# Attention into two feed-forward layers on one core: another order of the front's turns, the first weight blocks later, the eleventh unit pooled later

## The chip, the core and the metric

The kernel runs on one core of a Trainium2 chip. TensorE (PE) does the matrix products, VectorE (DVE), ScalarE (ACT) and GpSimd (POOL) the element-wise work, and SyncE (SP) issues most of the DMAs. The five engines run their own instruction lists in order and wait for each other through semaphores. The metric is the device time of one launch in microseconds (us), lower is better.

## The reference, cut to what matters

```python
# q, k, v: batch 4, heads 8, seq 576, head_dim 64
k_p = k.reshape(B, H, Sp, 8, D).mean(axis=3)         # keys and values pooled by 8
v_p = v.reshape(B, H, Sp, 8, D).mean(axis=3)
scores = scale * np.matmul(q, k_p.transpose(0, 1, 3, 2))
attn = softmax(scores)                               # over the 72 pooled keys
x = (attn @ v_p) as (2304 tokens, 512)
x = f1(x @ w_in) @ w_out                             # 512 -> 2048 -> 512, f1 a piecewise square
x = softplus(x @ w2_in) @ w2_out                     # the same sizes
```

## The kernel before

The attention is cut into 16 units, one for a pair of heads of a batch entry. The first ten (0 to 9, `FIRST = 10`) are done in the front, before the feed-forward layers; the other six are spread over the first products of layer 1. The products of the layers run in fp32r with each operand split into a high and a low part, three matmuls for each block. The rest of the program, from about 76 us on, is a nearly unbroken row of these matmuls on PE.

A unit passes through these steps in the front, and the text uses the short names on the left:

- **TQ(u)** on PE: six transposes of q (L1155) and two small matmuls that transpose and pair the keys (L1161), into PSUM banks 0 and 1. ACT then copies qT and kT out (`copy_qk`, L652 and L655). There is one qT and one kT buffer, so the copy of unit u waits until the scores of all units before u are done (`wait(act, scored, 2 * u)`).
- **S(u)** on PE: ten matmuls for the scores (L1178). DVE takes maxima and subtracts them (`take_max` L911, `shift` L918), ACT takes the exponential (`exp_scores` L661).
- DVE sums the exponentials (L934), inverts the sums (L939) and multiplies (L946): the softmax weights of unit u.
- **TP(u)** on PE: two groups of five transposes of the weights, h = 0 and h = 1 (L1199). ACT copies each group out (`copy_p`, L668 and L669). The group h = 1 of unit u waits until the results of all units before u have been stored (`wait(pe, x_stored, u)`), since it uses the same PSUM bank.
- **A(u)** on PE: the product with v (L1215). It waits for the weights' copies and for `v_summed`, the last pooling step of v on DVE (`sum_v`, L899). ACT stores the result in X (`store_x`, L674).
- POOL does the other pooling steps of k and v (`pool_keys` L553 and L559, `pool_values` L538 and L541).

Each engine's program is written out by hand as a loop over turns. In turn i of the front PE does S(i+1), TQ(i+2), A(i-2), TP(i-1), in this order; ACT does `copy_qk(i+2)`, `store_x(i-2)`, then the copies of TP(i-1) and the exponentials of unit i+1. DVE's turn i (`turn` in the vector block) is: sums of unit i, maxima of unit i+1 with the inversion of the sums between them, the two subtractions for unit i+1, weights of unit i, and last `sum_v(i-1)`.

After turn 8 PE does A(7), TP(8), A(8), TP(9) and A(9), and between them the first two blocks of layer 1's product, `make_h(0, 0)` and `make_h(0, 1)`, which are made in four chunks c0 to c3 of six matmuls each (L1263). The chunk c needs piece c of X split into high (ACT, L744) and low part (POOL L594 for pieces 0 and 1, DVE L992 for 2 and 3), and the weight block 0 split likewise (`hi_w` on ACT, L759; `lo_w(0, 0)` on POOL, L601). The third block, `make_h(0, 2)`, begins at 76.04 us in the profiled execution; from there on PE hardly waits.

SP loads k, q and v of each unit (288 KB each) and, between them, the weight blocks (`load_weights`, L439).

Of the kernel before, what the change touches and what calls it, by code (L numbers as in the profile page):

```python
# [38 lines left out]
FIRST = 10  # L39
# [23 lines left out]
PIECES = 4  # L63
# [22 lines left out]
LATE = FIRST - 2  # L86
# [4 lines left out]
def build(nc, q, k, v, w1_in, w1_out, w2_in, w2_out, out):  # L91
    with ExitStack() as ctx:
# [66 lines left out]
        def k_of(u):  # L159
            return k_one[:, 0, 4 * HD:6 * HD]  # L160
# [127 lines left out]
        def fill_done(n, piece):  # L288

            if n == 0:  # L290
                return (fill_lo_pool, piece + 1) if piece < FIRST_BY_POOL else (fill_lo_dve, piece - FIRST_BY_POOL + 1)
            if n in LO_BY_POOL:
                return fill_lo_pool, FIRST_BY_POOL + PIECES * LO_BY_POOL.index(n) + piece + 1
            before = n - 1 - sum(1 for m in LO_BY_POOL if m < n)
            return fill_lo_dve, PIECES - FIRST_BY_POOL + PIECES * before + piece + 1
# [113 lines left out]
        def _(sp):  # L409

            def load_k(u):
                wait(sp, k_paired, u - 3)
                sp.dma_start(k_in(u), k_src[u]).then_inc(k_loaded[u % PAIRS], 16)
# [17 lines left out]
            def load_weights(layer, k):  # L431

                n, slot = layer * JJ + k, W_ORDER[layer][k]
                if k >= 2:
                    sp.wait_ge(*w_done(layer, W_ORDER[layer][k - 2]))
                elif layer == 1:
                    sp.wait_ge(t_added, 4)
                for f in range(2):
                    sp.dma_start(w_raw[:, n % 2, f, :].rearrange("p (c j) -> p c j", c=KC),  # L439
                                 win_src[layer][slot + JJ * f]).then_inc(w_loaded[n % 2], 16)  # L440
# [43 lines left out]
            for u in range(3, FIRST):  # L484
                load_k(u)
                load_q(u)
                load_v(u - 2)
                if u >= LATE:
                    load_weights(0, u - LATE)
            for u in range(FIRST - 2, FIRST):  # L490
                load_v(u)
            load_shared(FIRST)
            load_weights(0, 2)
# [32 lines left out]
        def _(pool):  # L526
# [22 lines left out]
            def pool_keys(u):  # L549
                x = k_in(u)  # L550
                if u < FIRST:
                    pool.wait_ge(k_loaded[u % PAIRS], 16 * (u // PAIRS + 1))
                    nc.gpsimd.tensor_tensor(x[:, :, 0:4 * HD], x[:, :, 0:4 * HD], x[:, :, 4 * HD:8 * HD],  # L553
                                            ALU.add).then_inc(k_halved, 1)
                    pool.wait_ge(k_halved, u + 1)
                    wait(pool, qk_transposed, u - 1)
                    two, one = (x[:, :, r * 2 * HD:(r + 1) * 2 * HD].rearrange("p h (r d) -> p h r d", r=2)
                                for r in range(2))
                    nc.gpsimd.tensor_tensor(k_pair[:, u % 2, :, :].rearrange("p r (h d) -> p h r d", h=2), two, one,  # L559
                                            ALU.add).then_inc(k_paired, 1)  # L560
                else:
                    pool_sums(u, k_in(u), (k_one_loaded, 16 * (u - FIRST + 1)), k_halved, k_paired)
                    last_sum(u, k_in(u), k_of(u).rearrange("p (h d) -> p h d", h=2), k_paired, k_pooled)

            def pool_values(u):
                if u < FIRST:
                    pool_sums(u, v_in(u), (v_loaded[u % PAIRS], 16 * (u // PAIRS + 1)), v_halved, v_paired)
                else:
                    pool_sums(u, v_in(u), (v_one_loaded, 16 * (u - FIRST + 1)), v_halved, v_paired)
                    last_sum(u, v_in(u), v_in(u)[:, :, 0:HD], v_paired, v_pooled)  # L570
# [19 lines left out]
            def fill_lo_piece(n, piece):  # L590

                pool.wait_ge(fill_hi, PIECES * n + piece + 1)
                (data, source), = x_parts(n, piece)
                nc.gpsimd.tensor_tensor(xs[n % 2][:, 1, data], source, xs[n % 2][:, 0, data].bitcast(F32),  # L594
                                        ALU.subtract).then_inc(fill_lo_pool, 1)

            def lo_w(layer, k):

                n, slot = layer * JJ + k, W_ORDER[layer][k]
                pool.wait_ge(w_hi, n + 1)  # L600
                nc.gpsimd.tensor_tensor(W[:, slot, :, 1, :], w_raw[:, n % 2, :, :], W[:, slot, :, 0, :].bitcast(F32),  # L601
                                        ALU.subtract).then_inc(w_lo_pool, 1)
# [16 lines left out]
                                        ).then_inc(s_added, 1)  # L619

            pool_values(FIRST - 3)
            lo_w(0, 0)
            pool_values(FIRST - 2)
            fill_lo_piece(0, 0)
            pool_values(FIRST - 1)
            fill_lo_piece(0, 1)
            pool_keys(FIRST)
            pool_values(FIRST)
            for layer in range(2):
# [13 lines left out]
        def _(act):  # L643
# [19 lines left out]
            def copy_p(u, h):  # L663

                bank = p_bank(u, h)
                act.wait_ge(p_transposed, 2 * u + h + 1)
                a = NS_A * SSTEP
                nc.scalar.activation(pT_of(u, h)[:, 0:a], ps[0:SP, bank, 0:a], ACT.Copy)  # L668
                nc.scalar.activation(pT_of(u, h)[:, a:S], ps[0:SP, bank + 1, 0:S - a], ACT.Copy).then_inc(p_copied, 1)  # L669
# [8 lines left out]
            def turn(i):  # L678

                if i <= FIRST - 3:  # L680
                    copy_qk(i + 2)
                if 2 <= i:
                    store_x(i - 2)
                if 6 <= i < 6 + PIECES:
                    fill_hi_piece(0, i - 6)
                for h in range(2):
                    if 1 <= i <= FIRST:
                        copy_p(i - 1, h)
                    if i <= FIRST - 2:
                        exp_scores(i + 1, h)  # L690
                if 5 <= i < 7:
                    hi_w(0, i - 5)

            def load_shared_qk(u):

# [51 lines left out]
            def hi_w(layer, k):  # L747

                n, slot = layer * JJ + k, W_ORDER[layer][k]
                act.wait_ge(w_loaded[n % 2], 32 * (n // 2 + 1))  # L750
                if layer == 0 and slot >= 3:
                    act.wait_ge(x_stored, FIRST)
                elif layer == 1 and slot in (2, 3):
                    act.wait_ge(step_done, 6 * NT)
                elif layer == 1 and slot >= 4:
                    act.wait_ge(t_lo, 2 * PRODUCTS)
                elif layer == 1:
                    act.wait_ge(step_done, STEPS)
                nc.scalar.activation(W[:, slot, :, 0, :], w_raw[:, n % 2, :, :], ACT.Copy).then_inc(w_hi, 1)  # L759
# [80 lines left out]
            for layer in range(2):  # L840
# [32 lines left out]
                for m in range(1, STEPS + 2):  # L873
# [6 lines left out]
                    p, i = divmod(m - 2, NT)  # L880
# [261 lines left out]
        def _(pe):  # L1142
# [75 lines left out]

            def turn(i):

                if i <= FIRST - 2:
                    score(i + 1)
                if i <= 0:
                    keep_warm(WARM[i + 1])
                if i <= FIRST - 3:
                    transpose_qk(i + 2)
                if 2 <= i:
                    attend(i - 2)
                if i >= 1:
                    for h in range(2):  # L1230
                        transpose_p(i - 1, h)

# [16 lines left out]
            def make_h(layer, a, chunks=range(KC)):  # L1249

                k, f = divmod(a, 2)
                n, fill, slot = layer * HPAIRS + a, fill_of(layer, k // JJ), W_ORDER[layer][k % JJ]
                banks, x = bank_pair(v_of_pair[n]), xs[fill % 2]
                for c in chunks:
                    if c == 0:
                        pe.wait_ge(*w_done(layer, slot))
                        pe.wait_ge(*banks_free(v_of_pair[n]))
                    if a % (2 * JJ) == 0:
                        pe.wait_ge(*fill_done(fill, c))
                    for s, (part, x_part) in enumerate(((0, 0), (1, 0), (0, 1))):  # L1260
                        for tb in range(2):
                            at = c * PIECE + tb * TB
                            last = mm(banks[:, tb, :], W[:, slot, f, part, c * P:(c + 1) * P], x[:, x_part, at:at + TB],  # L1263
                                      start=c == 0 and s == 0, stop=c == KC - 1 and s == 2)
                if KC - 1 in chunks:
                    last.then_inc(h_done, 1)
# [80 lines left out]
            make_h(0, 0, (2,))  # L1347
            for h in range(2):
                transpose_p(FIRST - 1, h)
            make_h(0, 1, (1,))  # L1350
            attend(FIRST - 1)
            make_h(0, 0, (3,))
            make_h(0, 1, (2, 3))
            for layer in range(2):
                for a in range(2 if layer == 0 else 0, HPAIRS):
                    make_h(layer, a)
# [32 lines left out]
```

## Time and profile before

| what | us |
|---|---|
| median of 3 timed runs | 867.46 (866.34 to 874.46) |
| profiled execution, own time | 862.46 |
| its span, first to last instruction | 860.7 |
| one turn of the front (36.18 to 41.05) | 4.87 |
| last scores of the front, S(9), end | 55.28 |
| `make_h(0, 2)` begins | 76.04 |

The span is 1.76 us shorter than the execution's own time, and the profiled execution is 5.0 us shorter than the median of the timed runs. PE is busy for 98% of the span, DVE for 69%, ACT for 57%, POOL for 42%. The page gives the busy time of each engine and the clock granted to PE in 40 slices of 21.5 us; the clock has two levels here, 2.4 GHz (1.00) and 1.2 GHz (0.50).

### The profile page before, as it was taken

To read this page: it belongs to the slowest core of one execution; us is meant where nothing else is said; L and a number is where in the kernel's file an instruction comes from. 1 tells how busy PE (TensorE), PEld (TensorE's weight loads), DVE (VectorE), ACT (ScalarE), POOL (GpSimd) and SP (SyncE) were. 2 spreads that over 40 slices of the span, in tenths; PEclk is the share of its full clock that TensorE was granted. 3 is DMA by queue.
4 is the path that set the end of the run, shared out by engine and by line. 5 is a ranking of instruction groups with operands and counts; after the bars stand their busy time and mean duration, and the time that the engine had idled before them with its cause. 6 is when DMAs were issued, how large, how long until landed. Compare 5 with 4: busy or idle time off the path is not lost.

```text
span 860.7 us, 13035 instructions
## 1 busy us (share of the span) xinstructions
PE 845.8 (98%) x5198; PEld 822.7 (96%) x5198; DVE 592.0 (69%) x618; ACT 490.5 (57%) x700; POOL 360.8 (42%) x290
## 2 busy tenths in 40 slices
PE   8989999999999999999999999999999899999998
PEld 7768999999999999999999999999999899999998
DVE  4983855532233598768657698898899989778642
ACT  3875665644445453444435868978887654445442
POOL 6994677744454600000000498888766500000000
PEclk9979999999999999999999999999999999999999
DMA  8952767565555896454633235675655698645532
GB/s 195 209 126 78 209 209 230 185 220 188 181 183 188 274 395 224 167 220 154 227 109 99 96 123 189 211 243 182 211 200 176 204 397 306 239 164 203 200 113 73
DMA packets 106539, 167.82 MB, mean 195 GB/s; under 512 B 21872, under 2 KB 94448, under 8 KB 101872
## 3 DMA queue, kind: packets, MB, share of 16 engines
q1 hardware_dynamic: 93800, 157.86, 54.9%
q10 hardware_dynamic: 12680, 9.14, 3.7%
q8 instruction: 41, 0.67, 0.3%
q14 instruction: 18, 0.15, 0.1%
HBM read 96.21 MB, written 70.78 MB: 194 GB/s over the span
## 4 chain that ended last, share of the span: by engine, by line
PE 84%; DVE 6%; ACT 3%; DMA 3%; SPq 1%; issue 1%; POOL 1%; ACTq 0%; DVEq 0%
PE ps L1263 41%; PE ps L1281 37%; DVE t_a L1052 2%; DMA ops<-gops 2%; PE ps L1178 1%; DVE ops L1064 1%; PE ps L1215 1%; DMA w_raw<-in_moe_w_in_dram 1%; PE ps L1296 1%; PE ps L1321 1%; PE ps L1199 1%; DVE xs L992 1%; ACT qT L652 1%; PE ps L1155 1%; DVE t_a L1055 1%
## 5 line engine op out<-in xcount | busy, mean ns | idle before, releaser
L1263 PE MATMUL ps<-xs,W 128*128 128x384 f32 x2304 | 408.2, 336 | 0.8 <-DVE ops L1044 0.8
L1263 PEld LDWEIGHTS ps<-xs,W 128*128 128x128 f32 x2304 | 399.3, 188 | 5.8 <-issue 4.9
L1281 PE MATMUL ps<-xs,Tm 128*128 128x384 f32 x1968 | 345.9, 336 | 3.4 <-DVE xs L992 3.0
L1281 PEld LDWEIGHTS ps<-xs,Tm 128*128 128x128 f32 x1968 | 342.2, 189 | 4.3 <-issue 3.5
L744 ACT ACTIVATE xs<-ops 128x768 fp32r<-128x768 f32 (+1 forms) x148 | 111.7, 826 | 159.1 <-PE ps L1281 149.9
L608 POOL TENSOR_TENSOR ops<-ops 128x384 f32<-128x384 f32 x48 | 72.9, 1519 | 303.2 <-DVE ops L1064 221.9
L992 DVE TENSOR_TENSOR xs<-ops,xs 128x768 fp32r<-128x768 f32 (+1 forms) x148 | 130.2, 941 | 1.8 <-ACT xs L744 1.8
L1044 DVE SCALAR_TENSOR_TENSOR ops<-ps,t_a 128x768 f32<-128x768 f32 x48 | 45.9, 956 | 110.4 <-ACT t_a L768 110.2
L766 ACT ACTIVATE t_a<-ps 128x768 f32<-128x768 f32 x48 | 39.0, 812 | 96.2 <-PE ps L1263 96.2
L1077 DVE TENSOR_TENSOR X<-ps,X 128x768 f32<-128x768 f32 x41 | 38.7, 955 | 77.8 <-PE ps L1281 77.8
L1064 DVE TENSOR_TENSOR ops<-t_a,t_b 128x768 f32<-128x768 f32 x48 | 62.8, 1308 | 19.7 <-ACT t_b L787 17.9
L1052 DVE SCALAR_TENSOR_TENSOR t_a<-t_b,t_a 128x768 f32<-128x768 f32 x48 | 71.4, 1487 | 1.1 <-ACT t_b L782 1.1
L618 POOL TENSOR_TENSOR ops<-ops 128x384 f32<-128x384 f32 x48 | 63.7, 1327 | 3.8
L615 POOL TENSOR_TENSOR ops<-ops 128x384 f32<-128x384 f32 x48 | 64.1, 1335 | 0.0
L610 POOL TENSOR_TENSOR ops<-ops 128x384 f32<-128x384 f32 x48 | 56.1, 1170 | 0.0
L775 ACT ACTIVATE t_a<-ps 128x768 f32<-128x768 f32 x48 | 38.8, 809 | 30.0 <-DVE ops L1064 24.7
L787 ACT ACTIVATE t_b<-t_b 128x768 f32<-128x768 f32 x48 | 40.2, 838 | 12.5 <-DVE t_a L1052 12.5
L1055 DVE SCALAR_TENSOR_TENSOR t_a<-ps,t_a 128x768 f32<-128x768 f32 x48 | 46.0, 958 | 1.7
L744 ACT ACTIVATE xs<-X 128x768 fp32r<-128x768 f32 x46 | 37.4, 836 | 10.9 <-PE ps L1281 7.1
L992 DVE TENSOR_TENSOR xs<-X,xs 128x768 fp32r<-128x768 f32 x36 | 40.7, 1155 | 1.9 <-ACT xs L744 1.9
L777 ACT ACTIVATE t_a<-t_a 128x768 f32<-128x768 f32 x48 | 40.7, 848 | 1.6
L768 ACT ACTIVATE t_a<-t_a 128x768 f32<-128x768 f32 x48 | 40.6, 847 | 1.5
(88 smaller groups left out, 650.6 us busy)
## 6 DMA issues: line engine op xcount, KB each, us to landing
gops<-ops SPq DMA_DIRECT2D x48, 1344.0 KB, 5.8
ops<-gops SPq DMA_DIRECT2D x36, 1536.0 KB, 6.8
X<-gops SPq DMA_DIRECT2D x22, 384.0 KB, 6.4
w_raw<-in_moe_w_in_dram SPq DMA_DIRECT2D x32, 256.0 KB, 3.9
t_raw<-in_moe_w_out_dram SPq DMA_DIRECT2D x6, 1024.0 KB, 10.0
out_dram<-y_out ACTq DMA_DIRECT2D x11, 384.0 KB, 2.6
k_raw<-in_k_dram SPq DMA_DIRECT2D x10, 288.0 KB
q_raw<-in_q_dram SPq DMA_DIRECT2D x20, 144.0 KB, 7.6
```

The source lines that it names most:

```text
L608: nc.gpsimd.tensor_tensor(ops[:, slot, S1, :], ops[:, slot, G21, :], ops[:, slot, G22, :], ALU.add).then_inc(s_added, 1)
L610: nc.gpsimd.tensor_tensor(ops[:, slot, S3, :], ops[:, slot, G11, :], ops[:, slot, G21, :], ALU.subtract).then_inc(s_added, 1)
L615: nc.gpsimd.tensor_tensor(ops[:, slot, S2, :], ops[:, slot, S1, :], ops[:, slot, G11, :], ALU.subtract).then_inc(s_added, 1)
L618: nc.gpsimd.tensor_tensor(ops[:, slot, S4, :], ops[:, slot, G12, :], ops[:, slot, S2, :], ALU.subtract).then_inc(s_added, 1)
L744: last = nc.scalar.activation(xs[n % 2][:, 0, data], source, ACT.Copy)
L992: last = nc.vector.tensor_tensor(xs[n % 2][:, 1, data], source, xs[n % 2][:, 0, data].bitcast(F32), ALU.subtract)
L1044: nc.vector.scalar_tensor_tensor(out=g, in0=bank_pair(v_of_pair[a]), scalar=1.0, in1=t_a[:, a % 2, :, :], op0=ALU.max, op1=ALU.min).then_i ...
L1052: nc.vector.scalar_tensor_tensor(out=u, in0=b, scalar=1.0, in1=u, op0=ALU.subtract, op1=ALU.subtract).then_inc(r_made, 1)
L1055: nc.vector.scalar_tensor_tensor(out=u, in0=bank_pair(v_of_pair[n]), scalar=0.0, in1=u, op0=ALU.max, op1=ALU.subtract).then_inc(s_made, 1)
L1064: nc.vector.tensor_tensor(g, t_a[:, a % 2, :, :], t_b[:, a % 2, :, :], ALU.add).then_inc(g_made, 1)
L1263: last = mm(banks[:, tb, :], W[:, slot, f, part, c * P:(c + 1) * P], x[:, x_part, at:at + TB], start=c == 0 and s == 0, stop=c == KC - 1 a ...
L1281: last = mm(banks[:, d, :], Tm[:, t, part, j, d * P:(d + 1) * P], g[:, g_part, at * TB:(at + 1) * TB], start=at == 0 and s == 0, stop=at = ...
```

## The change

PE's turns from turn 1 on go TQ(i+2), A(i-2), S(i+1), TP(i-1): the scores move behind the product with v. ACT takes both copies of TP(i-1) before both exponentials, and splits the weight blocks 0 and 1 at the end of turns 7 and 8 and not of 5 and 6. SP loads weight block 0 after v of unit 7 and block 1 after v of unit 8. POOL pools v of unit 8 ahead of the weight block's low part, and waits for the last low piece of X on DVE before it pools unit 10. At the end of the front, chunk c3 of `make_h(0, 0)` goes ahead of A(9), and c1 of `make_h(0, 1)` behind it.

```diff
@@ SP
-                if u >= LATE:
-                    load_weights(0, u - LATE)
-            for u in range(FIRST - 2, FIRST):
+            for u in range(LATE, FIRST):
+                load_weights(0, u - LATE)
                 load_v(u)
@@ POOL
             pool_values(FIRST - 3)
+            pool_values(FIRST - 2)
             lo_w(0, 0)
-            pool_values(FIRST - 2)
             fill_lo_piece(0, 0)
             pool_values(FIRST - 1)
             fill_lo_piece(0, 1)
+            pool.wait_ge(*fill_done(0, PIECES - 1))
             pool_keys(FIRST)
@@ ACT, turn
                 for h in range(2):
                     if 1 <= i <= FIRST:
                         copy_p(i - 1, h)
+                for h in range(2):
                     if i <= FIRST - 2:
                         exp_scores(i + 1, h)
-                if 5 <= i < 7:
-                    hi_w(0, i - 5)
+                if LATE <= i + 1 <= LATE + 1:
+                    hi_w(0, i + 1 - LATE)
@@ PE, turn
-                if i <= FIRST - 2:
+                if i <= 0:
                     score(i + 1)
-                if i <= 0:
                     keep_warm(WARM[i + 1])
                 if i <= FIRST - 3:
                     transpose_qk(i + 2)
                 if 2 <= i:
                     attend(i - 2)
                 if i >= 1:
+                    score(i + 1)
                     for h in range(2):
                         transpose_p(i - 1, h)
@@ PE, end of the front
-            make_h(0, 1, (1,))
+            make_h(0, 0, (3,))
             attend(FIRST - 1)
-            make_h(0, 0, (3,))
-            make_h(0, 1, (2, 3))
+            make_h(0, 1, (1, 2, 3))
```

On PE, one turn of the front and the start of the next stood like this before (TQ is the first two rows, A the third, TP the next four, S the one after):

```order
L1155 MATMUL ps<-ident,q_raw 128x96 x6
L1161 MATMUL ps<-ident,k_pair 128x72 x2
L1215 MATMUL ps<-pT,v_sum 64x288 x4
L1199 MATMUL ps<-ident,prob 72x115 x4
L1199 MATMUL ps<-ident,prob 72x116
L1199 MATMUL ps<-ident,prob 72x115 x4
L1199 MATMUL ps<-ident,prob 72x116
L1178 MATMUL ps<-kT,qT 116x72 x10
```

With the change, the same place on PE (line numbers are one higher):

```order
L1156 MATMUL ps<-ident,q_raw 128x96 x6
L1162 MATMUL ps<-ident,k_pair 128x72 x2
L1216 MATMUL ps<-pT,v_sum 64x288 x4
L1179 MATMUL ps<-kT,qT 116x72 x10
L1200 MATMUL ps<-ident,prob 72x115 x4
L1200 MATMUL ps<-ident,prob 72x116
L1200 MATMUL ps<-ident,prob 72x115 x4
L1200 MATMUL ps<-ident,prob 72x116
```

The scores stand between the product with v and the transposes of the weights, and no longer ahead of the transposes of q and k.

On POOL, the end of the front stood like this before (v_raw is v of units 7, 8 and 9, W the weight block's low part, xs the low pieces of X, k_one the keys of unit 10):

```order
L538 TENSOR_TENSOR v_raw<-v_raw 72x2x256
L541 TENSOR_TENSOR v_raw<-v_raw 72x2x128
L601 TENSOR_TENSOR W<-w_raw,W 128x2x512
L538 TENSOR_TENSOR v_raw<-v_raw 72x2x256
L541 TENSOR_TENSOR v_raw<-v_raw 72x2x128
L594 TENSOR_TENSOR xs_55<-X,xs_55 128x768
L538 TENSOR_TENSOR v_raw<-v_raw 72x2x256
L541 TENSOR_TENSOR v_raw<-v_raw 72x2x128
L594 TENSOR_TENSOR xs_55<-X,xs_55 128x768
L538 TENSOR_TENSOR k_one<-k_one 72x2x256
```

With the change, the same place on POOL (line numbers are one lower):

```order
L537 TENSOR_TENSOR v_raw<-v_raw 72x2x256
L540 TENSOR_TENSOR v_raw<-v_raw 72x2x128
L537 TENSOR_TENSOR v_raw<-v_raw 72x2x256
L540 TENSOR_TENSOR v_raw<-v_raw 72x2x128
L600 TENSOR_TENSOR W<-w_raw,W 128x2x512
L593 TENSOR_TENSOR xs_55<-X,xs_55 128x768
L537 TENSOR_TENSOR v_raw<-v_raw 72x2x256
L540 TENSOR_TENSOR v_raw<-v_raw 72x2x128
L593 TENSOR_TENSOR xs_55<-X,xs_55 128x768
L537 TENSOR_TENSOR k_one<-k_one 72x2x256
```

The weight block's low part now follows v of unit 8, and the wait ahead of the last row is new.

## Rows read from the trace of the kernel before

**Rows 1.** The page: clock granted to PE by slice; a group, busy us and mean ns.

```profile
PEclk9979999999999999999999999999999999999999
...
L744 ACT ACTIVATE xs<-X 128x768 fp32r<-128x768 f32 x46 | 37.4, 836 | 10.9 <-PE ps L1281 7.1
```

**Rows 2.** Windows: PE, PEld, DVE, ACT, POOL busy us (instructions), PE clock, DMA.

```profile
36.18:41.05 4.87, 4.65 (x50) 3.47 (x49) 4.45 (x10) 3.83 (x11) 4.71 (x5) 1.00 0.98 211
...
49.97:51.97 2.00, 0.00 (x0) 0.00 (x1) 2.00 (x4) 1.97 (x6) 2.00 (x2) 0.75 1.03 208
51.97:55.28 3.31, 3.28 (x27) 2.82 (x29) 1.69 (x2) 2.73 (x7) 3.23 (x3) 0.50 1.02 216
...
75.25:76.04 0.79, 0.01 (x1) 0.03 (x1) 0.64 (x1) 0.79 (x2) 0.00 (x0) 1.00 0.00 0
...
685.50:689.20 3.70, 1.65 (x10) 1.36 (x9) 3.70 (x4) 0.41 (x1) 3.62 (x4) 1.00 0.97 295
689.30:692.70 3.40, 3.40 (x13) 3.40 (x12) 3.18 (x5) 3.06 (x5) 1.03 (x1) 0.50 1.12 423
```

**Rows 3.** Timeline of ACT at the stall: start, us, instruction, idle before and releaser.

```profile
49.17 1.06 ACT L759 ACTIVATE W<-w_raw 128x1024 fp32r<-128x1024 f32 x1 [1.15 <-DMA w_raw<-in_moe_w_in_dram]
50.13 0.67 ACT L652 ACTIVATE qT<-ps 128x288 f32<-128x288 f32 x1
...
51.17 0.68 ACT L674 ACTIVATE X<-ps 128x576 f32<-128x576 f32 x1
```

**Rows 4.** Timeline of PE over one turn.

```profile
40.46 0.66 PE L1199 MATMUL ps<-ident,prob 115*72 115x115 f32 x5 [0.22 <-ACT X L674]
41.05 1.24 PE L1178 MATMUL ps<-kT,qT 64*116 64x72 f32 x20
42.22 0.71 PE L1155 MATMUL ps<-ident,q_raw 96*128 96x96 f32 x6
...
43.29 1.19 PE L1215 MATMUL ps<-pT,v_sum 72*64 72x288 f32 x8
44.41 0.29 PE L1199 MATMUL ps<-ident,prob 115*72 115x115 f32 x1
```

**Rows 5.** Timeline of DVE over one turn.

```profile
43.22 0.53 DVE L911 TENSOR_REDUCE pmax<-ps 116x5 f32<-116x360 f32 x1
...
45.05 0.90 DVE L946 TENSOR_TENSOR prob<-prob,den 116x720 f32<-116x720 f32 x1
45.86 0.81 DVE L899 TENSOR_TENSOR v_sum<-v_raw 72x128 f32<-72x128 f32 x1
```

**Rows 6.** The weights' product and the last step of v, by line: ns min/median/max.

```profile
L946 DVE TENSOR_TENSOR prob<-prob,den x10: 896/1104/2725, 16.2 to 63.4; 116x720 f32<-116x720 f32 x10
...
L899 DVE TENSOR_TENSOR v_sum<-v_raw x10: 278/814/1368, 22.2 to 66.1; 72x128 f32<-72x128 f32 x10
```

**Rows 7.** Timeline of PE at turn 1.

```profile
17.90 1.24 PE L1178 MATMUL ps<-kT,qT 64*116 64x72 f32 x20 [0.64 <-ACT qT L652]
```

**Rows 8.** Timeline of the end of the front: ACT's exponential, POOL, three chunks on PE.

```profile
41.84 0.51 ACT L661 ACTIVATE prob<-prob 116x360 f32<-116x360 f32 x1
...
48.71 2.36 POOL L601 TENSOR_TENSOR W<-w_raw,W 128x1024 fp32r<-128x1024 f32 x1
...
55.50 1.26 POOL L538 TENSOR_TENSOR v_raw<-v_raw 72x512 f32<-72x512 f32 x1
...
57.53 1.82 POOL L594 TENSOR_TENSOR xs<-X,xs 128x768 fp32r<-128x768 f32 x1
...
71.86 3.39 PE L1263 MATMUL ps<-xs,W 128*128 128x384 f32 x18
```

**Rows 9.** Timeline of PE where its clock was 0.50.

```profile
53.07 2.21 PE L1178 MATMUL ps<-kT,qT 64*116 64x72 f32 x20
...
55.22 2.19 PE L1215 MATMUL ps<-pT,v_sum 72*64 72x288 f32 x8
...
57.33 2.14 PE L1199 MATMUL ps<-ident,prob 115*72 115x115 f32 x10
```

## Prediction

> **What bounds the kernel now.** The clock line of the page comes first: one weak slice, near the start [rows 1]. From 76 us on PE waits for next to nothing and the change alters nothing there, so the question is when `make_h(0, 2)` begins: at 76.04 before, when PE's stand of 0.79 us ends [rows 2]. Next, the windows. In a middle turn of the front PE is busy 4.65 of 4.87 us, DVE 4.45 and POOL 4.71 [rows 2]: three engines are nearly full, and PE sets the pace. Then the place where this breaks: PE stands still from 49.97 to 51.97, and in the stretch that follows the clock granted to it is 0.50, the lower of its two levels [rows 2]. ACT's timeline says why. ACT waits 1.15 us for the second weight block, splits it for 1.06 us, and only then copies q and k of unit 9 and stores the result that TP(6) waits for [rows 3]. This stall, and the clock it costs, is what the later loads and splits take away. Two figures to keep: S(9) ends at 53.07 + 2.21 = 55.28 [rows 9], and from there to 76.04 it is 20.76 us.
>
> **Loads and splits, a gain.** Without the stall S(9) would begin two turns behind the S at 41.05 [rows 4], at 50.8, and end at 52.0: 3.3 us earlier. At the high clock A, TP and the chunk behind them would save about half of their 2.2 us each [rows 9], some 3 us. c3 ahead of A(9) lets ACT begin on `make_h(0, 0)` sooner, which is worth most of the stand of 0.79 us. Together about 7 us, if the turns keep their 4.87. The loads themselves cost nothing: k, q and v of unit 9, 864 KB, now go ahead of block 0, 4.1 us at the 211 GB/s of rows 2, and the splits come two turns, 9.7 us, later. Without that cover the 1.15 us of rows 3 would come back and grow by what is missing.
>
> **The new order of PE's turn, a loss.** The same matmuls are issued, so PE's 4.65 us of work stay; what changes is what each waits for. Two chains that were open close into rings.
>
> First ring, through ACT. `copy_qk(i+2)` waits for S(i+1), because there is one qT buffer, and ACT runs it ahead of `store_x(i-2)`, for which the second half of TP(i-1) waits. Before, S(i+1) was long done by then. Now one turn is S 1.24 [rows 4], copies and store 1.72 (50.13 to 51.85 [rows 3]), hand-over to PE 0.12 (51.85 to 51.97 [rows 2, 3]), second half of TP 0.59 (40.46 to 41.05), TQ 1.07 (42.22 to 43.29), A 1.12 (43.29 to 44.41) [rows 4], and then the next S: 5.86 us, and 5.9 with the hand-over from S to ACT, at most that 0.12 too and put at 0.05.
>
> Second ring, through DVE. A(i-2) waits for `sum_v(i-2)`, the last item of DVE's turn i-1, which starts with the maxima of S(i). Before, S(i+1) and TQ ran in between; now S(i+1) stands behind A(i-2). So S 1.24, DVE from the maxima at 43.22 to the end of `sum_v` at 46.67, 3.45 [rows 5], A 1.12: 5.81 us, 5.9 with two hand-overs. Two terms of it vary. The product with the weights took 0.90 in that turn and 1.10 in the median; `sum_v` took 0.81, its median, and 0.28 at best [rows 6]. What they wait for is POOL, whose nearest row is an operation of 1.26 us [rows 8]: one whole operation ahead of each gives 5.9 - 0.53 + 2.52 = 7.9, none gives 5.4, and there the first ring decides. So a turn costs 5.9 to 7.9 us, and I take 5.9 + 0.2 = 6.1, by the medians of rows 6.
>
> Both copies ahead of both exponentials on ACT cost nothing: DVE's sum needs both exponentials, and the pair ends at the same place.
>
> In turn 1 TQ(3) now goes first at 17.90, where S(2) stood [rows 7], takes 1.07, and S(2) ends at 17.90 + 1.07 + 1.24 = 20.2. Seven turns lead from S(2) to S(9): 20.2 + 7 x 6.1 = 62.9, against 55.28: **+7.6 us**. The bounds are +6.2 (turns of 5.9) and +20 (7.9).
>
> **The end of the front.** Let Z be the end of S(9). ACT splits block 0 at the end of turn 7: S(8) ended at Z - 6.1, then come 0.05 + 1.72, a split of a piece of X, 0.84 [rows 1], the rest of a turn, 1.89 (40.46 to the end of the exponential at 42.35 [rows 4, 8]), and 1.06 [rows 3]: done at Z - 0.5. POOL has pooled v of unit 8 by then and stands waiting; it takes 2.36 for the low part, 1.82 for piece 0, 2.03 for v of unit 9 (55.50 to 57.53) and 1.82 for piece 1 [rows 8]: Z + 7.5. Behind that PE has c1, TP(8), c0, A(8), c2, TP(9), c3, A(9) and three more chunks: seven chunks at 3.39/3 = 1.13 [rows 8], two A at 1.12 and two TP at half of 2.14 [rows 9], 12.3 us. `make_h(0, 2)` begins at Z + 19.8, or up to 1.2 us later where POOL waits for DVE. That is 20.4 in the middle against 20.76 before, and I count it at nothing. POOL's new wait puts unit 10's six pooling steps, at most 1.3 us each alone [rows 8], behind the last low piece, which I put at Z + 11 (c1 at Z + 7.5 and the splits of the last piece); TQ(10) comes one block of four chunks, 4.5 us, after Z + 20.4, so they end at Z + 19 and are covered, and cost only what they overrun Z + 25.
>
> At the high clock throughout, the sum is +7.6: 862.46 + 7.6 = 870.1 for the profiled execution, and for the median, which lies 5.0 above it, 867.46 + 7.6 = 875.1.
>
> **The clock.** In the first ring PE stands still once a turn, from the end of TP's first half to ACT's store: 0.05 + 1.72 + 0.12 - 0.6 = 1.3 us. Before, it stood 0.22 [rows 4]. In this trace the clock fell after a stand of 2.00 us, and again at 689 us, after a stretch of 3.70 us in which PE worked 1.65; it did not fall for the stand of 0.79 us [rows 2]. 1.3 us lies between, comes seven times, and grows where A waits for `sum_v`; I expect falls. A turn at 1.2 GHz costs, in the first ring, S 2.21, A 2.19, half a TP 1.07 [rows 9], TQ doubled to 2.14, and ACT's 0.05 + 1.72 + 0.12: 9.5 us, 3.4 more than 6.1. The first fall lasted from 51.97 to beyond 57.33 [rows 2, 9], most of such a turn, the second 3.4 us [rows 2]. I take 2.5 of the seven turns at the low clock: +8.5.
>
> The Trainium skill, in "TensorE: Matmul & The Clock Gate", section "Why this matters for your kernels", ties a fall to gaps between bursts of matmuls that are longer than any counted here; by that rule the clock stays up in the turns and the time is case B's. The fall after 2.00 us speaks against it.
>
> **The rivals.**
> A, the forecast: both rings, and the low clock in about 2.5 turns: 867.46 + 7.6 + 8.5 = **883.6**. One to four such turns give 878 to 889. Chance 0.38.
> B, both rings, the clock stays up in the turns: 875.1, and 873.7 (turns of 5.9) to 882 (6.9). For it: no stand reaches 2 us by the median rows. Chance 0.27.
> C, both rings, and the clock, once down, stays down until the dense chunks: six turns, 6 x 3.4 = 20.4 more, 895.5, from 890 to 899. For it: after 51.97 PE worked without pause, and TP at 57.33 still took 2.14 [rows 9]. Against it: the second fall was over after 3.4 us [rows 2]. Chance 0.22.
> D, the other side: the rings are no longer than the old turn, the turns stay at 4.87 and the stall is gone: 867.46 - 7 = 860.5. It decides where 20.2 + 7t falls under 55.28, at a turn t of 5.0 us; DVE's 3.45 would have to shrink to 2.5 and ACT's 1.72 to 0.8. Against it: rows 3 and 5 give these times for work that waits for nothing but POOL. Chance 0.08.
> E, the stall's gain and the turns' loss cancel, with turns near 5.4: within 5 us of 867. Chance 0.05.
>
> **How the numbers follow.** Within about 1% (8.7 us) a change can hardly be told from none. Faster by more, under 858.8, is the tail of D: 0.03. Slower by more, over 876.1, is A and C and half of B: 0.73. The rest is 0.24. The range takes in B from its lower bound, A, and C but for its upper tail, and leaves out D, most of E and a little more: 872 to 897.
>
> **What would show it.** In the changed trace: some 6 us between the starts of S; ACT's first copy of q released by S (L1179) and not by the keys' matmuls; PE idle for over 1 us ahead of TP's second half, behind ACT's store (L674); A right behind `sum_v`; clock 0.50 for longer than before ahead of 80 us; no wait of ACT for a weight block. It is wrong if the turns stay under 5.0 us or S(9) ends before 57; its clock term is wrong if PE's clock stays at 1.00 through the turns.

## The result

| | us |
|---|---|
| before, median of 4 runs beside it | 866.90 (866.17 to 874.46) |
| after, median of 4 runs | 896.20 (888.41 to 899.08) |
| ratio | 1.0335, 95% interval 1.0299 to 1.0372 |
| after, profiled execution, own time and span | 899.08 and 897.2 |

The change makes the kernel 29.3 us slower. Two of the four executions took 898.67 and 899.08 us (the second is the profiled one), two took 888.41 and 893.73. Ratios here and below leave out executions over 1.5% longer than the fastest of their kernel, so that a median and its ratio can differ a little.

In the profiled execution all of the loss lies ahead of unit 10. S(9) ends at 89.30 + 2.21 = 91.51 against 55.28 [rows 9], 36.2 us later. From there to TQ(10) it is 25.44 us (to 116.95, shown below) against 25.00 before:

```profile
80.28 0.66 PE L1155 MATMUL ps<-ident,q_one 96*128 96x96 f32 x6
```

One turn on PE, from S to S (compare rows 4):

```profile
44.19 2.21 PE L1179 MATMUL ps<-kT,qT 64*116 64x72 f32 x20
...
48.42 1.15 PE L1200 MATMUL ps<-ident,prob 115*72 115x115 f32 x5 [0.91 <-ACT X L674]
49.36 1.17 PE L1156 MATMUL ps<-ident,q_raw 96*128 96x96 f32 x6
...
51.27 2.19 PE L1216 MATMUL ps<-pT,v_sum 72*64 72x288 f32 x8
```

The turn takes 9.20 us, not 4.87, and every matmul takes as long as at the low clock in rows 9: S 2.21, A 2.19. The page's clock line does not show this (it reads 9 from the first slice on, and the windows of the front give 1.00); the durations do, and S(0) already took 2.21:

```profile
8.97 2.21 PE L1179 MATMUL ps<-kT,qT 64*116 64x72 f32 x20
```

```profile
5.50:17.00 11.50, 11.43 (x66) 10.79 (x66) 2.30 (x5) 3.23 (x8) 8.60 (x9) 1.00 0.98 212
```

From 5.58 to 38.30 PE worked 32.68 of 32.72 us, with durations of the low clock throughout. So in this execution the clock was low before a ring first made PE stand (0.91 us, up to 39.22). In the turn above ACT and DVE (compare rows 3 and 5):

```profile
46.54 0.69 ACT L652 ACTIVATE qT<-ps 128x288 f32<-128x288 f32 x1 [4.65 <-PE ps L1179]
...
49.09 0.28 DVE L900 TENSOR_TENSOR v_sum<-v_raw 72x128 f32<-72x128 f32 x1
```

ACT now waits for S (L1179) before it copies q, and PE's second half of TP waits 0.91 us for ACT's store behind these copies. The chain of waits of this stretch goes round exactly that way, turn after turn (start, us, what):

```profile
44.26 2.19 PE ps L1179 x20
...
46.54 0.69 ACT qT L652
...
47.80 0.49 ACT X L674
...
53.46 2.19 PE ps L1179 x20
```

That is the first ring: S, the copies and the store on ACT, half of TP, TQ, A, S. `sum_v` was done at 49.37, 1.9 us before A, so the second ring does not decide here. The sums of waits of this execution from 20 to 120 us (engine and line waiting, for what: us in all, times, longest) name the two new waits of the change:

```profile
ACT qT L652 <- PE ps L1179: 31.6, 7, 4.6
POOL W L600 <- ACT W L760: 15.1, 1, 15.1
```

No wait of ACT for a weight block is left. At the end of the front, POOL, DVE and PE, and a window there (columns as in rows 2):

```profile
93.56 2.25 PE L1264 MATMUL ps<-xs,W 128*128 128x384 f32 x6
...
94.97 2.57 DVE L900 TENSOR_TENSOR v_sum<-v_raw 72x128 f32<-72x128 f32 x1
...
95.60 1.79 POOL L593 TENSOR_TENSOR xs<-X,xs 128x768 fp32r<-128x768 f32 x1
...
97.64 1.19 PE L1216 MATMUL ps<-pT,v_sum 72*64 72x288 f32 x8 [1.83 <-issue]
...
116.95 0.66 PE L1156 MATMUL ps<-ident,q_one 96*128 96x96 f32 x6
```

```profile
99.10:102.50 3.40, 3.40 (x17) 3.17 (x15) 3.33 (x7) 1.98 (x4) 0.73 (x1) 0.50 0.00 0
```

The clock comes up between c0 (2.25 us at 93.56) and A(7) (1.19 at 97.64), and falls once more for 3.4 us behind a stand of 1.83 us, in which `sum_v` took 2.57 us and POOL's piece of X ran beside it.

### The profile page after: what moved, and what is told of

Same layout as the page of the kernel before. It is cut to its first block, busy times and chain, and to the rows that moved or that the text cites. A ratio compares the mean times of both kernels' runs of the same rounds, so it can differ in the third digit from the quotient of the medians.

```text
span 897.2 us, 13036 instructions
## 1 busy us (share of the span) xinstructions
PE 878.6 (98%) x5198; PEld 849.4 (95%) x5198; DVE 589.9 (66%) x618; ACT 491.0 (55%) x700; POOL 353.1 (39%) x290
## 4 chain that ended last, share of the span: by engine, by line
PE 89%; DVE 4%; ACT 3%; DMA 2%; issue 1%; POOL 1%; SPq 0%; ACTq 0%; DVEq 0%
PE ps L1264 40%; PE ps L1282 35%; PE ps L1179 3%; PE ps L1216 3%; PE ps L1200 2%; DVE t_a L1053 2%; DMA ops<-gops 1%; PE ps L1156 1%; DVE ops L1065 1%; PE ps L1329 1%; PE ps L1297 1%; PE ps L1162 1%; PE ps L1322 1%; ACT qT L652 1%; DVE t_a L1056 1%
```

## The experiments

The theory: the loss is PE's new order, by its two rings, and the stands that the rings bring keep the clock low. Rivals: the later loads and splits cost it; any order without S at the head of the turn costs it; the clock is low by itself, whatever the order. Every run stands against runs of the kernel before on the same chip.

**1. The order alone.** The kernel before with nothing but the hunk "PE, turn" of the change:

```diff
-                if i <= FIRST - 2:
+                if i <= 0:
                     score(i + 1)
...
                 if i >= 1:
+                    score(i + 1)
                     for h in range(2):
```

> The kernel before with only the new order in PE's turns; loads, splits, ACT's and POOL's order as before. Theory R (two rings on PE's turn, made longer by the low clock): nearly the whole loss is here, 888 to 900 us, turns of 9.2 us at the low clock, ACT's first copy of q released by the scores. Rival L (the later loads, splits and pooling cost it): within 5 us of before, 862 to 872, turns of 4.9 us.

887.45 us (885.79 to 898.32) against 866.65; ratio 1.0266 (1.0191 to 1.0341). PE's timeline in its profile, and a window:

```profile
24.66 1.19 PE L1215 MATMUL ps<-pT,v_sum 72*64 72x288 f32 x8 [1.92 <-DVE v_sum L899]
25.78 1.62 PE L1178 MATMUL ps<-kT,qT 64*116 64x72 f32 x20
...
29.42 1.15 PE L1199 MATMUL ps<-ident,prob 115*72 115x115 f32 x5 [0.91 <-ACT X L674]
...
34.39 2.21 PE L1178 MATMUL ps<-kT,qT 64*116 64x72 f32 x20
...
43.60 2.21 PE L1178 MATMUL ps<-kT,qT 64*116 64x72 f32 x20
```

```profile
26.40:34.39 7.99, 7.08 (x43) 5.04 (x39) 4.67 (x8) 3.81 (x10) 7.70 (x8) 0.50 0.71 179
```

Here the clock was up at the start. The second ring made PE stand 1.92 us in front of the first A, the clock fell in the S behind it, and from then on the first ring turned at 9.2 us. So the order alone brings most of the loss, 20.8 of 29.3 us (0.55 us under the range expected). In this profile the mean granted clock over the records is 0.965; the two shorter executions of after have 0.965 and 0.958, the two longer ones 0.998, so the same course, up and then down, is likely in the shorter ones (they were not profiled).

**2. Everything but the order.** The kernel after with that hunk taken back.

> The changed kernel with the scores back at the head of PE's turn; all else of the change stays. Theory R: the rings are open, turns of 4.9 us, ACT no longer waits for a weight block, and the 7 us of the stall and its low clock are gained: 858 to 863. Rival L: 885 to 900.

868.51 us (865.53 to 872.21); ratio 1.0025 (1.0001 to 1.0049). The loss of the change is gone, but the gain isn't there. POOL, PE and a window:

```profile
54.34 2.36 POOL L600 TENSOR_TENSOR W<-w_raw,W 128x1024 fp32r<-128x1024 f32 x1 [3.95 <-ACT W L760]
```

```profile
51.30 1.24 PE L1179 MATMUL ps<-kT,qT 64*116 64x72 f32 x20
...
59.28 2.26 PE L1264 MATMUL ps<-xs,W 128*128 128x384 f32 x6 [3.68 <-POOL xs L593]
```

```profile
59.20:64.00 4.80, 4.38 (x14) 2.55 (x14) 4.73 (x6) 0.29 (x1) 4.72 (x3) 0.50 0.09 26
```

S(9) does come earlier, at 51.30 against 53.07, and ACT waits for no block. The time misses the expected 858 to 863: the split of block 0 now stands at the end of ACT's turn 7; POOL waits 3.95 us for it, so its low part begins at 54.34 and not at 48.71 [rows 8], PE stands 3.68 us in front of the first chunk, and the clock falls there. TQ(10) begins at 83.42, 3.1 us later than before.

**3. The scores between TQ and A.** After with the turn TQ, S, A, TP:

```diff
+                if i >= 1:
+                    score(i + 1)
                 if 2 <= i:
                     attend(i - 2)
                 if i >= 1:
-                    score(i + 1)
                     for h in range(2):
```

> The changed kernel with the scores between the key transposes and the product with v: TQ, S, A, TP. Theory R: what closes the rings is that S stands behind A; here copy_qk runs beside A and A(i-2) no longer stands ahead of S(i+1), so the turn is about 5 us and the time 858 to 866. Rival T (it is TQ ahead of S that hurts, through the one qT buffer): turns stay at 6 to 9 us and the time at 880 or more.

869.68 us (864.87 to 873.23); ratio 1.0034 (1.0008 to 1.006). Turns take 4.79 us, as expected; the time misses the expected 858 to 866, since the stand in front of the first chunk (3.66 us) is that of run 2. So for the turns it isn't S's leaving the head of the turn that costs, it is S behind A.

**4. The stand filled.** After, with eight matmuls of 128 rows by 32 columns between the halves of TP, work added whose result is thrown away:

```diff
                     score(i + 1)
-                    for h in range(2):
-                        transpose_p(i - 1, h)
+                    transpose_p(i - 1, 0)
+                    for _ in range(8):
+                        mm(ps[96:P, 4, 0:P], ident[:, 96:P], ident[:, :], start=True, stop=True)
+                    transpose_p(i - 1, 1)
```

> The changed kernel with eight small matmuls of 128 columns (128 rows, 32 columns of the array, result thrown away) in PE's stand between the two halves of TP, about 1.2 us of work at the high clock. Theory R with the clock: PE has no stand left, the clock stays at 1.00 in the turns, turns of 6.0 to 6.2 us, 872 to 880, which is the price of the rings alone. Rival K (the low clock has another cause than the stand): the clock stays at 0.50, the extra work lengthens the turn to 9.2 to 10.5 us, 895 to 905.

878.38 us (873.99 to 885.36); ratio 1.0134 (1.008 to 1.0188): 18 us under after, though it does more work. A turn and its window:

```profile
33.13 1.24 PE L1179 MATMUL ps<-kT,qT 64*116 64x72 f32 x20
...
34.92 1.93 PE L1233 MATMUL ps<-ident 128*32 128x128 f32 x16
36.78 0.69 PE L1200 MATMUL ps<-ident,prob 115*72 115x115 f32 x5
...
75.69 1.31 PE L1266 MATMUL ps<-xs,W 128*128 128x384 f32 x6 [1.98 <-POOL xs L593]
```

```profile
33.13:39.89 6.76, 6.39 (x67) 5.25 (x65) 5.08 (x8) 3.83 (x10) 6.52 (x7) 1.00 0.59 135
```

In this profile the clock stays at 1.00, even behind a stand of 1.98 us at the end of the front, and the turns take 6.3 to 7.0 us. From the start of S to the second half of TP it is 36.78 - 33.13 = 3.65 us, 0.52 more than the first ring's own 3.13 by the prediction's rows and 0.39 more than the 3.26 of run 6 at the high clock (27.89 to 31.15), so seven turns carry 3.6 or 2.7 us of the added matmuls. S(9) ends at 66.85, 11.6 us later than before; less these it is +8.0 to +8.9, an estimate of the price of the rings at the high clock.

**5 to 7. One ring opened, the other, both.** After, with ACT's store ahead of the copies (5), with `sum_v(i-1)` at the head of DVE's turn (6), with both (7). PE's order is untouched in all three:

```diff
@@ ACT, turn (5 and 7)
+                if 2 <= i:
+                    store_x(i - 2)
                 if i <= FIRST - 3:
                     copy_qk(i + 2)
-                if 2 <= i:
-                    store_x(i - 2)
@@ DVE, turn (6 and 7)
+                if old and u >= 1:
+                    sum_v(u - 1)
                 if old:
...
-                    if u >= 1:
-                        sum_v(u - 1)
```

> The kernel after, with ScalarE's store_x(i-2) put ahead of copy_qk(i+2) in each turn: the store of the X tile, which releases the second half of TP, no longer stands behind the copies that need the new qT. Two rings is the theory: this opens the first (transposes, qT copy, X store, TP, next transposes) and leaves the second (A, sum_v on VectorE, next A). Then the turns are shorter than 9.20 us even if the clock stays low, about 5.8 to 6.8 us at full clock, the stand in front of A behind sum_v is what is left, and the kernel takes 870 to 888 us, still above before (866.9). Rival, one ring only: the second ring never decides, the turns return to 4.9 us and the time is that of the kernel with S at the head, 864 to 871. Rival, the clock by itself: the order doesn't matter, the clock stays low whatever ScalarE does, and it takes 890 to 899 as after does.

> The kernel after, with VectorE's sum_v(i-1) put at the head of its turn, ahead of the work on the new scores: A's operand no longer waits for the softmax of the score that TensorE issues behind it. By the theory of two rings this opens the second ring alone; the first, through ScalarE's qT copies and the X store, is the longer one at the low clock and stays, so turns of 9.2 us at the low clock, 5.8 to 6.6 at full clock, and 885 to 899 us if the clock is low in the front as in after, 873 to 882 if it is up. Rival, sum_v is what keeps PE waiting: turns of 4.9 us and 864 to 871 us.

> Both of these edits in the kernel after, with TensorE's order (TQ, A, S, TP) untouched. Two rings: with both open the order of TensorE costs nothing, turns are 4.8 to 5.2 us at full clock, and the time is that of the kernel after with S at the head of the turn, 864 to 872 us, the stand of 3.7 us in front of the first dense chunk included. Rival, the order itself (TQ next to A next to S on TensorE, its banks, or a third ring) is what costs: turns stay at 5.8 us or more and the time above 875.

| run | us | ratio |
|---|---|---|
| 5, first ring open | 884.15 (882.04 to 885.9) | 1.0208 (1.0154 to 1.0262) |
| 6, second ring open | 887.52 (884.25 to 897.83) | 1.0235 (1.017 to 1.03) |
| 7, both open | 871.2 (865.26 to 881.19) | 1.0038 (1.0007 to 1.007) |

All three came out where the two rings put them. What PE waits for says which ring is left. Run 5, a turn and a window; run 6, a turn at either clock; run 7 (its profile is of an execution of 881.19 us, left out of the ratio, in which the clock came up only at 48.7 us):

```profile
39.00 1.24 PE L1179 MATMUL ps<-kT,qT 64*116 64x72 f32 x20
...
44.22 1.19 PE L1216 MATMUL ps<-pT,v_sum 72*64 72x288 f32 x8 [1.37 <-DVE v_sum L900]
45.34 1.24 PE L1179 MATMUL ps<-kT,qT 64*116 64x72 f32 x20
```

```profile
46.68:56.92 10.24, 9.91 (x59) 8.04 (x58) 6.55 (x14) 5.44 (x15) 6.52 (x6) 0.50 0.57 135
```

```profile
27.89 1.24 PE L1179 MATMUL ps<-kT,qT 64*116 64x72 f32 x20
...
33.78 1.24 PE L1179 MATMUL ps<-kT,qT 64*116 64x72 f32 x20
...
37.04 1.14 PE L1200 MATMUL ps<-ident,prob 115*72 115x115 f32 x5 [1.40 <-ACT X L674]
42.01 2.21 PE L1179 MATMUL ps<-kT,qT 64*116 64x72 f32 x20
...
51.21 2.21 PE L1179 MATMUL ps<-kT,qT 64*116 64x72 f32 x20
```

```profile
50.47 1.24 PE L1179 MATMUL ps<-kT,qT 64*116 64x72 f32 x20
...
55.41 1.24 PE L1179 MATMUL ps<-kT,qT 64*116 64x72 f32 x20
```

With the first ring open, A waits for `sum_v` turn after turn and a turn takes 6.34 us at the high clock (39.00 to 45.34); the clock falls and rises several times. With the second open, the first ring alone takes 5.89 us at the high clock (27.89 to 33.78), where the prediction put 5.9; behind a stand of 1.40 us the clock falls, and its 9.2 us are back. With both open a turn takes 4.94 us in the same order on PE. So the order costs through these two rings and through nothing else that is as large, and neither ring alone is the cause: with one opened 18.0 and 21.4 us of the loss are left, with both 5.1.

**8. The splits one turn earlier.** Run 2's kernel (S at the head) with blocks 0 and 1 split at the end of turns 6 and 7:

```diff
-                if LATE <= i + 1 <= LATE + 1:
-                    hi_w(0, i + 1 - LATE)
+                if LATE <= i + 2 <= LATE + 1:
+                    hi_w(0, i + 2 - LATE)
```

> The kernel after with S at the head of the turn again (the second run's kernel, 868.51 us), and ScalarE's splits of weight blocks 0 and 1 one turn earlier, at the end of turns 6 and 7 in place of 7 and 8 (the blocks had landed at 44.9 and 48.4 us there, turn 6 ends at about 48.4). If the gain of the later loads was eaten by GpSimd's wait of 3.95 us for the split block, that wait goes, the low part is done at about 52.7 in place of 56.7, the stand of 3.68 us in front of the first chunk goes to under 1, the clock doesn't fall there, and the kernel takes 859 to 865 us, faster than before. Rival: the split then costs turn 7 and 8 on ScalarE what it saves on GpSimd, or GpSimd's next piece is the last one anyway, and it stays at 866 to 870.

865.79 us (863.87 to 889.04); ratio 0.9989 (0.9959 to 1.0019), against 1.0025 for run 2. POOL's wait is down to 0.57 us and the stand in front of the first chunk is gone, as expected, yet no gain is clear of noise. A new stand has taken their place, and the clock falls behind it (POOL, DVE and PE; A's 2.19 us is its time at the low clock):

```profile
56.22 2.48 POOL L593 TENSOR_TENSOR xs<-X,xs 128x768 fp32r<-128x768 f32 x1
...
56.95 1.90 DVE L900 TENSOR_TENSOR v_sum<-v_raw 72x128 f32<-72x128 f32 x1
...
58.99 2.19 PE L1216 MATMUL ps<-pT,v_sum 72*64 72x288 f32 x8 [1.55 <-DVE v_sum L900]
```

`sum_v`, 0.28 us when nothing is in its way, took 1.90: it ended at 58.85, just after POOL's piece of X (58.70). Even so, this profile takes 60.19 us from S(2) to TQ(10) (22.74 to 82.93) against 62.38 before (17.90 to 80.28). A gain of that size lies within the interval, but its loads also had 4.8 us more ahead of S(2), where the clock came up later, so it isn't shown.

**9 and 10. Only block 1 later.** The kernel before, its block 1 split at the end of turn 7 in place of 6; and the same with run 3's order:

```diff
-                if 5 <= i < 7:
-                    hi_w(0, i - 5)
+                if i in (5, 7):
+                    hi_w(0, (i - 5) // 2)
```

> The kernel before with one move on ScalarE: the split of weight block 1 at the end of turn 7 in place of turn 6, while block 0 keeps its split at the end of turn 5 and so GpSimd its early low part. The wait of ScalarE for the landing of block 1 was what stopped TensorE for 1.9 us and was followed by the fall of the clock at 51.97 us. Theory: the prediction's gain of about 7 us was real, and the change lost it because it also moved block 0, whose low part GpSimd needs at 48.7 us; then this kernel has no wait for a block in turn 6, S(9) starts at about 50.8 to 51.3 in place of 53.07, and it takes 859 to 864 us against 866.5. Rival: the stand only moves, to the first chunk or to a wait for sum_v in turn 8, since GpSimd and VectorE end the front anyway: 865 to 868.

> The same kernel with TensorE's turn as TQ, S, A, TP (S ahead of A, where both rings were open and a turn took 4.79 us in place of 4.87). If turns are all that counts beside the stand, eight turns give another 0.6 us: 858 to 864 us. Rival: A behind S comes later and holds up the last turns as in the third run, where the gain of the turns was not seen: the same as the kernel without this edit, or up to 2 us more.

867.15 us (863.46 to 889.31), ratio 1.0014 (0.9989 to 1.0039); and 867.04 (863.14 to 884.99), ratio 1.0014 (0.999 to 1.0038). Both miss the gain; the rivals' times came out. In run 10's profile a turn took 4.78 us where the clock was up (39.04 to 43.82), but behind a stand of 0.81 us, which ended at 25.13, it was low for two turns. In run 9 ACT waits for no block, but:

```profile
51.52 2.36 POOL L601 TENSOR_TENSOR W<-w_raw,W 128x1024 fp32r<-128x1024 f32 x1
...
51.83 2.83 DVE L946 TENSOR_TENSOR prob<-prob,den 116x720 f32<-116x720 f32 x1
...
56.07 1.85 PE L1215 MATMUL ps<-pT,v_sum 72*64 72x288 f32 x8 [1.45 <-DVE v_sum L899]
```

DVE's product with the weights, 0.90 us alone, stands until POOL's low part is done at 53.88 and ends 0.78 later; `sum_v` is late by it, PE stands 1.45 us, and the next S takes 2.21. The Trainium skill, "SBUF — State Buffer", section "Who interferes with whom", says that a VectorE operation with two inputs in SBUF and a GpSimd operation that reads SBUF exclude each other, and that whichever issues second waits for the whole of the first; the ends in runs 8 and 9 agree with it. In run 9's profile S(2) began at 24.31 and not at 17.90, but POOL's low part only 2.81 us later than before, so the two met at another place of the turn than in the trace of before; whether the edit alone would bring them together isn't shown.

**11. The change repaired.** Run 7 with run 8's earlier splits.

> The kernel after with its own TensorE order, both rings opened (ScalarE's X store ahead of the qT copies, sum_v at the head of VectorE's turn) and the two block splits one turn earlier. If order, rings and the late low part are the whole story, this is the change repaired: 2 to 6 us under the run with both rings open alone (871.2 us), so 864 to 869 us. Rival: the order keeps a cost of its own in executions whose clock comes up late (turns of 8.1 us at the low clock were seen with both rings open), and it stays at 870 to 874 us.

867.41 us (860.6 to 868.51); ratio 1.0018 (0.9994 to 1.0042). With both rings open and the low part in time, the change's order is as fast as the kernel before, and no faster; its turns:

```profile
31.95:36.88 4.93, 4.54 (x50) 3.52 (x49) 4.28 (x8) 3.83 (x10) 4.77 (x5) 1.00 0.93 206
```

**12. The clock held up.** Run 9 with ten matmuls of run 4's kind, again thrown away, ahead of A in turns 7 and 8.

> The kernel before with block 1 split at the end of turn 7 (the ninth run's edit) and 10 matmuls of 128 rows by 32 columns, whose result is thrown away, ahead of A in turns 7 and 8, where TensorE stood 1.45 us behind sum_v and the clock then fell for about 8.5 us. If what the front still pays is the fall of the clock behind such a stand, the clock stays up, the added matmuls cost under 1 us beyond the stand in each turn, and the kernel takes 860 to 865 us against 865.7. Rival: the clock's fall is replaced by the time of the added matmuls, or falls at another stand, and it stays at 865 to 868.

865.28 us (861.85 to 867.16); ratio 0.9983 (0.9961 to 1.0006). Turn 7 in its window:

```profile
50.06:57.22 7.16, 6.94 (x69) 5.57 (x68) 6.35 (x10) 4.73 (x12) 5.03 (x4) 1.00 0.45 114
```

The clock no longer falls, but the turn takes 7.16 us, 2.3 more than 4.87, so that what was won goes into the added matmuls. The time can't be told from the kernel before's, and no run here is faster than that kernel by more than its interval.

## Why the prediction was right, and where a size was off

**"The new order of PE's turn": right.** Both rings are there, and runs 5 to 7 show that each alone costs and that together they are the cost. At the low clock the first ring was put at 9.5 us and took 9.20 (S with the way through ACT 4.23 in place of 4.10, half a TP 0.94 in place of 1.07, TQ 1.91 in place of 2.14, A 2.12 in place of 2.19). At the high clock the first ring was put at 5.9 and took 5.89 (run 6), the second at 5.4 to 7.9 and took 6.34 and 6.60 (run 5; 39.00 to 45.34, 59.18 to 65.78); both together were put at +7.6, and run 4 gives +8.0 to +8.9.

**"The end of the front": right.** Counted at nothing, it was 25.44 against 25.00 us in after. POOL's new wait covered as said: k of unit 10 began at 101.77 and its pooling ended long before TQ(10).

**"The clock": the direction right, the term mis-sized.** The text took 2.5 of seven turns at the low clock, +8.5. Measured: 896.2 - 866.9 = 29.3 in all, less the 7.6 of the order, 21.7. In the profiled execution no turn ahead of 91 us was at the high clock. Its seven turns from S(2) to S(9) took 62.4 us (29.09 to 91.51) where 42.7 were counted, 19.7 more; another 8.9 were lost ahead of S(2), which ended at 29.09 and not 20.2, a part that the text had at the high clock throughout, as in the trace of before. Of a turn of 9.20 us the ring makes 1.10: run 7's turns at the low clock without a stand take 8.10 (35.80 to 43.90). The loss ahead of S(2) is in the main the execution's and not the change's: run 9, whose first turns are those of the kernel before, has 6.4 us of it, but there the clock was up at S(2), and the turns kept it up:

```profile
8.85 2.21 PE L1178 MATMUL ps<-kT,qT 64*116 64x72 f32 x20 [0.63 <-ACT qT L652]
...
24.31 1.24 PE L1178 MATMUL ps<-kT,qT 64*116 64x72 f32 x20 [0.63 <-ACT qT L652]
```

The low turns are the course of rival C (895.5). The step that failed is "2.5 of the seven turns at the low clock". It took the lengths of two falls [rows 2, 9] for that of a fall in the turns; both ended in stretches in which PE worked without pause, and each turn of the first ring has a stand of its own. The runs showed in its place: in run 1 the clock fell behind a stand, as foreseen (of the second ring, 1.92 us, and not of the first), and then stayed low through all the turns that were left, 61 us; in the profiled execution of after it did not fall but had never come up, and stayed low through all seven. Run 4, with the stand filled, had it up in all turns of its profile, which supports that the stands keep it low. How much of the 21.7 is owed to them isn't shown: one of the 29 executions of the kernel before beside runs 9 to 11 took 891.54 us with a mean clock of 0.998, much like after's two long ones, so a front at the low clock can come without the rings, and with four executions its share can't be taken out. By after's two shorter executions alone the change costs 21.5 and 26.8 us.

So it was in part luck that the number came out inside. The median lies 0.8 us under the upper end of 897, outside the 878 to 889 of the forecast A, and the four executions lie on both sides of it, two at 888 and 894 and two at 899, past the upper end.

The rule that the prediction cited from the Trainium skill ("TensorE: Matmul & The Clock Gate", section "Why this matters for your kernels") would have kept the clock up in the turns; run 1's fall behind a stand of 1.92 us, run 8's behind 1.55 and run 9's behind 1.45 speak against its rule, as rows 2 did.

**"Loads and splits, a gain": not there.** S(9) came 1.8 us earlier in run 2, where 2.3 were counted for its start, but the step left out that the block's later split also delays POOL's low part, in front of which PE stands 3.68 us. This term was not in the sum, but it priced the other side: rival D's 860.5 was not to be had with this change, since D's turns with the rest of it gave 868.51. In runs 8 and 9 a repair did not bring it either: with the stall gone from ACT, a stand behind `sum_v` took its place. Only the smallest part came: with c3 ahead of A(9) the stand of 0.79 us is gone (in after seven chunks follow each other from 109.22 without one, as in runs 2 and 8; in runs 9 and 12, which keep the old order there, it stays). The text also names the loads ahead of block 0 wrongly: they are k and q of unit 9 and v of unit 7, of the same size.

Of what was to show it, ACT's wait for S, the longer stretch at the low clock (by the durations; the records show 0.50 in run 1) and the missing wait for blocks came true; PE stood 0.91 us ahead of TP's second half, and over 1 us only at the high clock (1.40 in run 6); A right behind `sum_v` did at the high clock (runs 1, 4 and 5), not at the low one; 6 us between the starts of S only where the clock was up.

What stays open: why the clock comes up in some executions before S(0) and in others not until S(2), and in the profiled one of after not at all ahead of the chunks. And what would make this front faster: in the kernel before, DVE and POOL are so full that a stall which is taken away came back at another place in runs 2, 8 and 9, and run 12's interval includes no change.

## What to carry to other kernels

Before an instruction is moved behind another on one engine, follow what it releases on the others and back: where the way round returns to the same engine within a turn, the turn becomes the sum of that way, and where two such rings are closed, opening one takes back only a part. A turn with one short stand can cost twice, once for the stand and again for the clock, so price it at both levels of the clock, and do not take how long the clock was low in one stretch for how long it will be in another. Where three engines are over 90% busy, expect that a stall that is removed on one uncovers the next, as in runs 2, 8 and 9.

## What the runs showed of the hardware that was not expected

The clock can stay at 1.2 GHz for very long under steady work. In after it was low from S(0) on, though PE worked 32.68 of 32.72 us up to 38.30, and then through the turns with a stand of 0.91 us, in which PE worked 8.29 of 9.20 us. In run 1 it was low for 61 us (26.4 to 87.9), in the same turns. In both it came up only when these turns were over: in run 1 in the A behind S(9), TP and a chunk without a stand, in after by the A that came behind these three and a stand of 1.83 us. In run 7, whose turns at the low clock took 8.10 us without a stand, it came up at 48.7 us, amid the turns, then bore stands of 0.4 to 0.7 us a turn for 17 us, and fell behind one of 0.64. In run 4 it did not fall behind a stand of 1.98. So the length of the last stand alone did not tell in these runs whether the clock would fall:

```profile
43.90 2.21 PE L1179 MATMUL ps<-kT,qT 64*116 64x72 f32 x20
...
58.48 0.69 PE L1156 MATMUL ps<-ident,q_raw 96*128 96x96 f32 x6 [0.72 <-ACT qT L652]
...
65.16 1.63 PE L1216 MATMUL ps<-pT,v_sum 72*64 72x288 f32 x8 [0.64 <-ACT pT L669]
```
